# Attention over sparse scores, two expert layers: three engines' attention loops rolled up and one PSUM block moved

## The reference, cut to what matters

```python
# q, k, v: (4, 8, 576, 64) f32;  x: 2304 tokens of 512
scores = q @ k^T / 8
thresh = max(scores, -1) - tau
scores = where(scores >= thresh, scores, -1e9)
attn   = exp(scores - max); attn /= sum(attn) + 1e-9
x      = (attn @ v), as (2304, 512)
# then: one of 8 experts for each token (512 -> 1024 -> 512, relu, gate), and
# a dense layer 512 -> 2048 -> 512 with h * tanh(softplus(h))
```

## Time and profile before

| | |
|---|---|
| time, median of 3 runs (lowest to highest) | 1092.91 us (1092.45 to 1094.31) |
| the profiled execution: its time, its span | 1094.31 us, 1092.6 us |
| PE, DVE, ACT, POOL busy, share of the span | 95%, 58%, 46%, 53% |
| mean granted clock of TensorE | 0.975 |
| instructions recorded | 20910 |

### The profile page before, as it was taken

One profiled execution on the slowest core, in us unless ns is written; L12 is line 12 of the kernel. 1 busy time (PEld: TensorE's weight loads), 2 busy tenths in 40 slices (PEclk: granted clock), 3 DMA queues, 4 the chain that ended last, 5 costly groups with the idle time before them and its releaser, 6 DMA issues.

```text
span 1092.6 us, 20910 instructions
## 1 busy us (share of the span) xinstructions
PE 1033.4 (95%) x6712; PEld 858.3 (79%) x6712; DVE 629.5 (58%) x1455; ACT 504.7 (46%) x1019; POOL 583.7 (53%) x672
## 2 busy tenths in 40 slices
PE   7999999999949999799999985899999999999998
PEld 5777777777627887688888874799998999989997
DVE  6888888988653221121222124567767667676664
ACT  5777777777552222122222212354554545545553
POOL 3344344433348776776630606876556565565554
PEclk9999999999968999899999997999999999999999
DMA  8145432441267889888834507401001010010000
GB/s 210 45 114 166 118 98 61 118 128 52 78 208 226 284 245 305 284 274 292 279 120 184 173 20 212 116 11 58 1 1 59 1 58 0 0 58 0 30 1 29
DMA packets 97525, 128.84 MB, mean 118 GB/s; under 512 B 34400, under 2 KB 51808, under 8 KB 96928
## 3 DMA queue, kind: packets, MB, share of 16 engines
q1 hardware_dynamic: 72976, 67.32, 20.9%
q0 software_dynamic: 18880, 53.22, 15.6%
q10 hardware_dynamic: 5584, 7.16, 1.9%
HBM read 111.69 MB, written 15.99 MB: 117 GB/s over the span
## 4 chain that ended last, share of the span: by engine, by line
PE 59%; DMA 5%; POOL 5%; issue 2%; DVE 2%; ACT 1%; POOLq 0%; SPq 0%; ACTq 0%; DVEq 0%
PE ps L1048 18%; PE ps L1050 18%; PE ps L1049 18%; DMA stage<-w 4%; POOL wl L560 3%; PE ps L1074 1%; PE ps L1123 1%; PE ps L988 1%; PE ps L1044 1%; POOL wh L571 1%; DVE mn L1449 1%; PE ps L998 1%; POOL xs_far L597 0%; ACT junk L778 0%; DMA yg<-y_sorted,gidx 0%
## 5 line engine op out<-in xcount | busy, mean ns | idle before, releaser
L560 POOL TENSOR_TENSOR wl<-stage,wh 128x512 fp32r<-128x512 f32 x128 | 161.9, 1290 | 56.7 <-DMA stage<-w 52.3
L672 POOL TENSOR_TENSOR mg<-mw,mr 128x384 f32<-128x384 f32 x96 | 118.5, 1234 | 75.1 <-DVE mr L1468 75.0
L720 ACT ACTIVATE ex<-sc,rmin 128x576 f32<-128x576 f32 x144 | 111.6, 776 | 78.3 <-DVE sc L1244 78.3
L1048 PE MATMUL ps<-yth,winh 128*128 128x384 f32 x384 | 133.0, 346 | 8.8 <-DVE mw L1456 8.8
L676 POOL TENSOR_TENSOR gl<-mg,gh 128x384 fp32r<-128x384 f32 x96 | 97.6, 1016 | 78.3 <-ACT gh L847 78.3
L1050 PE MATMUL ps<-yth,winl 128*128 128x384 f32 x384 | 130.9, 341 | 0.0
L1049 PE MATMUL ps<-ytl,winh 128*128 128x384 f32 x384 | 130.6, 340 | 0.0
L1254 DVE SCALAR_TENSOR_TENSOR pm<-sc,thr,ex 128x576 f32<-128x576 f32 x144 | 116.2, 811 | 20.0 <-POOL thr L526 15.1
L1244 DVE TENSOR_SCALAR_CACHE_REDUCE sc<-ps,nscale 128x576 f32<-128x576 f32 x144 | 116.8, 813 | 10.2 <-PE ps L897 9.6
L526 POOL TENSOR_SCALAR thr<-rmin,taup 128x1 f32<-128x1 f32 x144 | 71.4, 497 | 85.0 <-DVE sc L1244 83.7
L1050 PE MATMUL ps<-wouth,gl 128*128 128x512 f32 x288 | 114.0, 396 | 0.0
(11 more groups left out here) (187 smaller groups left out, 2304.7 us busy)
## 6 DMA issues: line engine op xcount, KB each, us to landing
stage<-w SPq DMA_DIRECT2D x128, 256.0 KB, 4.6
wh<-w POOLq DMA_DIRECT2D x32, 1024.0 KB, 8.5
y_sorted<-yo ACTq DMA_DIRECT2D x25, 256.0 KB, 4.2
q_t<-qT SPq DMA_DIRECT2D x16, 288.0 KB, 3.6
k_t<-kT SPq DMA_DIRECT2D x16, 288.0 KB, 3.8
vb<-v SPq DMA_DIRECT2D x16, 288.0 KB, 4.5
out<-os SPq DMA_DIRECT2D x18, 256.0 KB, 4.2
stage<-w_in SPq DMA_DIRECT2D x16, 256.0 KB, 3.2
```

Source lines behind the costliest of these rows:

```text
L560: g.tensor_tensor(dst, raw, src.bitcast(F32), ALU.subtract).then_inc(w_split, 1)
L672: g.tensor_tensor(mg[:, f % 2, :], mw[:, f % 2, :], mr[:, f % 2, :], ALU.mult).then_inc(g_done, 1)
L720: act.activation(ex[:, i % 2, t * S:(t + 1) * S], sc[:, i % 2, t * S:(t + 1) * S], ACT.Exp, bias=rmin[:, i % 2, t:t + 1], scale=-1.0).then ...
L1048: pe.matmul(out_, lhs_h, rhs_h, start=start, stop=False)
```

## The change

Three things are done. The PSUM block of the transposed result, OUT0, moves behind OT0 in the last block. PE waits for the norm of the unit before ahead of each `weighted`, and the wait in the last three `turn_back` goes; `t_part(3)` now waits as its neighbours do. And on ACT, PE and DVE iterations 1 and 2 of the four become a hardware loop, with iterations 0 and 3 written out before and after; POOL and SP stay unrolled.

```diff
-    OUT0 = 1536 + S // 2
+    OUT0 = OT0 + P
...
# the same on act, pe and dve
-        for b in range(NITER):
-            attention(b, b == NITER - 1)
+        attention(0, False)
+        with act.Fori(1, NITER - 1) as b:
+            attention(b, False)
+        attention(NITER - 1, True)
...
# weighted
             pe.wait_ge(pt_ready, 2 * u + 2)
+            wait(pe, normed, u)
...
-        def turn_back(body, i, last):
+        def turn_back(body, i):
 
             u = unit(body, i)
-            if last and i + 3 >= ITER:
-                pe.wait_ge(normed, u)
             pe.wait_ge(ot_ready, u + 1)
...
# t_part
-            pe.wait_ge(normed, NUNIT if n == 3 else min(NUNIT, chunk_ready(k)))
+            pe.wait_ge(normed, min(NUNIT, chunk_ready(k)))
```

More of the change, by code:

```diff
@@ L961, in attention @@
                     scores(b, i + 3)
-                turn_back(b, i, last)
+                turn_back(b, i)
                 if not (last and i + 2 >= ITER):
@@ L975, in _ @@
         transpose(0, 1)
-        for b in range(NITER):
-            attention(b, b == NITER - 1)
+        attention(0, False)
+        with pe.Fori(1, NITER - 1) as b:
+            attention(b, False)
+        attention(NITER - 1, True)
         def t_part(n):
             k = n // RG
-            pe.wait_ge(normed, NUNIT if n == 3 else min(NUNIT, chunk_ready(k)))
+            pe.wait_ge(normed, min(NUNIT, chunk_ready(k)))
             if n >= 4:
@@ L1310, in _ @@
             mask(0, i, 1)
-        for b in range(NITER):
-            attention(b, b == NITER - 1)
+        attention(0, False)
+        with dve.Fori(1, NITER - 1) as b:
+            attention(b, False)
+        attention(NITER - 1, True)
         for n in range(0, RG * KD, 2):
```

## The result

The changed kernel takes 1101.36 us (median of 4 runs, 1099.86 to 1106.47) and the kernel before, on the same chip, 1093.37: a ratio of 1.0083 [1.0065, 1.010], slower by 0.8%. I had forecast 1097.6 us, so 3.8 too little, inside the range of 1093.8 to 1102.5. The profiled execution took 1101.55 us against 1094.31, its span grew from 1092.6 to 1099.9.

The account below looks back on a forecast made before the run. PE sets the attention's pace, VectorE close behind, with 0.11 us slack for the new wait. Regular 0.0, tails 0.9, late units 0.6, end 0.2, registers 0.5, jump 2.5 sum to 4.7 us: 1097.6 us, range 1093.8 to 1102.5.

Parts of the forecast that it names:

- rival 2: Attention: every unit pays 0.08 us, 5.8 more, giving 1103.4 us, or 1100.5 with half of it; chance 0.18.
- A regular unit pays nothing: PE's wait for norm ahead of weighted: slack 0.11 us minus latency 0.11, so 0.0.
- Tails: Every ninth unit's three-part norm delays the next weighted sum; 0.13 us stays for each of 7, 0.9 us.
- Late units and the end: Two units with VectorE late pay 0.30 us each, 0.6; the last weighted sum pays 0.2.
- The place of the transposed output: OUT0's move removes the wait in the last three turn backs; nothing gained.
- the released transposes: Transposes of x for n = 3 may start before the last norm; no gap there, nothing gained.
- Register work: Register operations in the attention's looped units on three engines: 0.5 us, between 0 and 2.9.
- The jump back: One jump per loop near 156 us may find code dropped: 2.5 us, between 0 and 3.9.
- a body of 6.5 packets: PE's attention loop body in 16 KB code packets, against 6.1 in the last stage; perhaps no longer resident.
- The upper bound of 3.9: Most the jump back was to cost, in us: a small transfer's time from issue to landing.
- shifts as a whole: Behind the attention, routing, gathers and expert loads, all started by the last norm, move by its whole delay.

Follow-up runs that it names:

- after: The changed kernel itself, with wait, moved OUT0 and loops, against the kernel before: 1101.36 us, ratio 1.0083.
- g: The kernel before with only the wait for the norm added, OUT0 in its old place, no loops: 1100.47 us, ratio 1.0051.
- a: The changed kernel with all three attention loops unrolled, new wait and moved OUT0 kept: 1099.56 us, ratio 1.0037 to the kernel before.
- j: The changed kernel without loops, the norm's wait put ahead of weighted's other two: 1096.62 us, ratio 1.0011 to the kernel before.
- d: The kernel before with hardware loops on PE and ScalarE only, VectorE unrolled: 1097.06 us, ratio 1.0014.
- b: The kernel before with the three hardware loops, no new wait, OUT0 in its old place: 1102.65 us, ratio 1.0062.
- c: The kernel before with the hardware loop on VectorE alone: 1105.73 us in one run, its profiled execution.
- l: The changed kernel with the norm's wait first and 60 idle waits before VectorE's wait for tau: 1097.34 us, ratio 1.0023 to the kernel before.
- k: The changed kernel with 180 further idle waits on VectorE ahead of the attention: 1106.88 us in one run, its profiled execution.
- e: The changed kernel with 36 idle waits on VectorE ahead of the attention: 1099.04 us, ratio 1.0052 to the kernel before.
- h: The changed kernel with 90 idle waits on VectorE ahead of the attention: 1099.17 us in one run, its profiled execution.
- i: The changed kernel with 36 idle waits on VectorE and the norm's wait first: 1096.62 us, ratio 1.0027 to the kernel before.
- f: The changed kernel, loops kept, with the norm's wait put first of weighted's waits: 1100.64 us, ratio 1.0062 to the kernel before.

## Why the prediction was right or wrong, step by step

**Kind and direction: right.** The time is lost in the attention, by the wait and by the jump; the forecast of slower held. That the time also came out near the forecast is in part luck. The attention lost twice what the sum had: the regular unit, put at 0.0, cost most of 3.0 us, and the jump, put at 2.5, cost 5.6. The terms put too high (tails, late units, end and registers) gave back about 1 us, and 1.7 us of the attention's delay don't show in the medians. The measured 1101.4 lies nearer to half of rival 2 (1100.5) than to the forecast.

**"A regular unit pays nothing": wrong, by 3.0 us.** The step took slack 0.11 minus latency 0.11. It had the form of the wait right, an instruction of its own on the queue, and the place to read its price too, the transposes' second half. But it read the price from the copy's end to the weights (159.83 to 159.94), while the slack was counted to a weighted sum whose weights and first matmul started together. The matmul of that group, in the kernel before, came later than its weights:

```profile
159.97 0.74 PE L916 MATMUL ps<-ident,pm 128*128 128x128 f32 x5
```

So such a wait cost 0.15 to the first matmul already there, and it costs 0.15 in after, g and a; 0.15 less 0.11 is the 0.04 of every unit. That the same wait, carried by the instruction, costs 0.05 and would have been hidden, I had not considered. The 3.0 us are what the order of the waits makes, with the 0.05 more in each tail. Rival 2 had the kind (every unit pays); its price was 0.08 a unit, the runs show 0.04.

**Tails: mechanism right, size about right.** A pair of units after a tail takes 8.50 us in j against 4.17 + 4.26 = 8.43 before: 0.07 each and 0.5 in seven, where I had 0.13 and 0.9: my 0.11 for the wait was 0.05 here. In after a pair takes 8.63, of which 0.13 belongs to the order of the waits above.

**Late units and the end: right.** The late norms of units 12 and 32 make the weighted sums of 13 and 33 later by 0.25 and 0.24 in j (I had 0.30 each), of which 0.21 and 0.19 stay; the end costs 0.1 (0.2). All of j's delay is 0.91 us, or 1.0 counted from its own start, against 1.7 for these terms.

**"The place of the transposed output" and the released transposes: right**, nothing for both together (g against a).

**Register work, 0.5: about half of it in after, and not where I had it.** The period is the same in unrolled and looped units everywhere, so the operations of every unit show no price. Without the wait the loops cost 0.04 us in d and at most 0.22 in b before the jump. With it, after loses 0.13 more than a in the first unit of the loop and 0.11 more at unit 33, which b and c lose there too. With the norm's wait first it is 0.3 in each pass's first unit (l against j).

**"The jump back", 2.5 us of 0 to 3.9: mis-sized, and PE was the wrong suspect.** From unit 35 to 39 after loses 5.84 us, less 0.27 that a loses there: 5.6 us. It is made of VectorE's stop, which leaves PE idle for 3.95, and of 1.58 for PE's two instruction groups at the lower clock: 5.5. VectorE's second pause of 1.41 falls under PE's slow scores, and k, without it, pays the same. My bounds took it that a jump can go to code that has to be loaded again; in the kernel before, nothing showed that. The stops show it for VectorE, with a load in each of them (163.40 us in after), and no run shows it for PE. Queue 8, whose loads of 16 KB are 53 in before and c and 47 in after and d, where PE has its loop, started 11 loads for 2784 of PE's instructions from 21.2 to 148.3 us of after, one for 253. It brought none between 148.3 and 236.6 us, over the jump and the whole second pass of PE's body of 1598 queue instructions (I had 1587), and none between 865.5 and 1026.7, over the jump and the second pass in the last stage. So my doubt about a body of 6.5 packets was idle. I never counted over how many blocks VectorE's lies, as its body of 335 instructions is a fifth of PE's. VectorE's loop in the last stage gave no warning: it has 282 instructions and goes on within 0.4 us of its branch, in before as in after. The upper bound of 3.9, a transfer's time, is close to the stop itself (4.1 and 4.0 in after and b). What I left out is that a stop has a second price, the clock of the engine that is kept waiting: 0.50 for 3.4 us here.

From VectorE's branch to its loop's next instruction it is 4.5 us in after. With loads of 8 KB for 128 instructions, 335 instructions over three of them jumped back without a stop (e, h, i, l) and over four they did not (after, b, c, f, k). How many blocks are held in all, no run here shows. My prediction counted PE's body in packets and not VectorE's: at 8 KB for 128 instructions that is 21 KB or 2.6 blocks, which can lie over three or over four.

**Behind the attention.** I said that the rest "shifts as a whole". Up to the router it does: its last matmul ends 13.8 us behind the last norm in every run but l. In medians the delay of the attention comes out again within 2 us: 3.9 late in a gives 4.3, 4.0 in g 5.2, 7.6 in b 7.4, 9.7 in after 8.0, 2.3 in l 2.0, but 0.0 in d 1.8. In single executions the expert stages move by several us either way, so whether after's missing 1.7 us is given back there or is spread of the runs, these runs don't tell.

**The sum, corrected.** Late units, tails and end 0.9 + order of the waits 3.0 + jump 5.6 + registers and start 0.2 = 9.7 us, which is the 9.68 seen. The first two are a's delay and the third is read from units 35 to 39, less a's; the last is 0.13 and 0.11 for the registers less 0.06 for an earlier start.

## What to carry to other kernels

When a wait is added to an instruction that already has some, the wait that will end last should be the one the instruction carries: it cost 0.05 us there and 0.15 as an instruction of its own, and with a slack of 0.11 the rest came back in every unit. Read such a price to the same instruction as the slack, here the first matmul and not its weights. When a large body is rolled into a loop, count for every engine, the small ones first, over how many loads of its code the body lies (8 KB and 128 instructions each on VectorE here), not only how long it is: shifting VectorE's body by 18 to 45 instructions took away a stop of 4 us and the drop of PE's clock behind it. Read single places of the trace (the end of a stage, less its start) where whole times scatter by more than the effect.

## What the hardware showed that I had not expected

- VectorE stopped for 4.2 to 4.5 us at a jump back to a body of 335 instructions that lay over four blocks of 128, and a second time for 1.4 to 2.3 us, 13 instructions later, when the entry was close to a block's end. With some 50 instructions left in the block (k) there was no second stop. SP's loads of q, k and v ran during the stop (287 GB/s in after's row). They don't make it (293 GB/s in l, no stop); whether they lengthen it wasn't tried.
- PE jumped back over 1598 instructions within 0.3 us (157.5 to 157.8 in after).
- After a stretch of 4.50 us in which PE was busy for 0.63 its granted clock fell to 0.50 (after), and stayed there for 3.4 us in after and k, and for 6.8 us in b, c and f.
- A wait as an instruction of its own on PE's queue cost 0.15 us from the norm's end to the first matmul (after, a, g), and 0.05 when the instruction carried it (j, f, l).
- Two waits that follow each other on VectorE's queue took one instruction (18 more on the page for 36 waits in e, 90 for 180 in k), and such instructions followed each other every 0.10 us.
